# Attention, Fourier mixing and two feed-forward layers on one core: tables in 128 rows, another order of loads, cheaper transposes, and layer 1's last slots spread over fifteen chunks

## What is computed

```python
def phi(x):                                   # q, k: [4, 4, 1088, 32], S1, S2: [8, 32]
    a = einsum('rd,bhsd->bhsr', S1, x); b = einsum('rd,bhsd->bhsr', S2, x)
    return einsum('bhsi,bhsj->bhsij', a, b).reshape(..., 64)
kv, z = einsum('bhsf,bhsd->bhfd', phi(k), v), phi(k).sum(tokens)
x = (phi(q) @ kv) / (phi(q) @ z + 1e-6)       # -> [4, 1088, 128]
mixed = real(fft(fft(x, axis=tokens), axis=channels))
u = x + mixed
un = (u - mean(u)) / sqrt(var(u) + 1e-6)
x2 = u + relu(un @ w_ch1) @ w_ch2             # layer 1
h = relu(x2 @ w_in)                           # layer 2
conv = sum over k of conv_w[k] * h[token + k - 1]
out = (h * sigmoid(conv)) @ w_out
```

## Time and profile before

| | |
|---|---|
| median of 3 runs | 354.21 us (353.78 to 357.87) |
| span of the profiled execution | 352.7 us |
| PE busy | 312.0 us (88%) |
| DVE busy | 213.8 us (61%) |
| ACT busy | 191.6 us (54%) |
| POOL busy | 45.1 us (13%) |
| mean granted TensorE clock | 0.821 of full |
| DMA | 12.69 MB, mean 36 GB/s |

### The profile page before, as it was taken

One profiled execution on the slowest core, in us unless ns is written; L12 is line 12 of the kernel. 1 busy time (PEld: TensorE's weight loads), 2 busy tenths in 40 slices (PEclk: granted clock), 3 DMA queues, 4 the chain that ended last, 5 costly groups with the idle time before them and its releaser, 6 DMA issues.

```text
span 352.7 us, 4540 instructions
## 1 busy us (share of the span) xinstructions
PE 312.0 (88%) x1644; PEld 273.0 (77%) x1644; DVE 213.8 (61%) x373; ACT 191.6 (54%) x361; POOL 45.1 (13%) x93
## 2 busy tenths in 40 slices
PE   8499999999995019999998999979999899999966
PEld 7499999999995019989998987667876677878733
DVE  1522362233450004776888576948669999999994
ACT  2121023115211003556766798867778898999962
POOL 0000000008000001332222243830000000000000
PEclk9755555555555558999999999989999999999999
DMA  6800900200302000000000000000000100100101
GB/s 199 269 3 15 296 2 18 69 27 26 82 27 81 27 24 2 0 2 0 4 0 3 0 3 0 0 2 0 1 2 0 63 2 0 63 0 3 64 0 63
DMA packets 4192, 12.69 MB, mean 36 GB/s; under 512 B 780, under 2 KB 1548, under 8 KB 4170
## 3 DMA queue, kind: packets, MB, share of 16 engines
q1 hardware_dynamic: 4170, 12.41, 10.9%
HBM read 10.18 MB, written 2.23 MB: 35 GB/s over the span
## 4 chain that ended last, share of the span: by engine, by line
PE 29%; DVE 17%; ACT 4%; POOL 3%; issue 1%; POOLq 0%; DVEq 0%; ACTq 0%
PE ps L549 7%; DVE arena L945 5%; DVE arena L938 5%; DVE arena L933 5%; PE ps L460 5%; PE ps L462 5%; PE ps L461 5%; PE ps L453 3%; PE ps L503 2%; PE ps L509 2%; ACT arena L654 1%; PE ps L476 1%; ACT arena L740 1%; POOL arena L341 1%; ACT arena L727 1%
## 5 line engine op out<-in xcount | busy, mean ns | idle before, releaser
L549 PE MATMUL ps<-arena,wout 128*128 128x364 f32 (+1 forms) x192 | 63.6, 470 | 3.4 <-DVE arena L945 3.3
L549 PEld LDWEIGHTS ps<-arena,wout 128*128 128x128 f32 x192 | 35.5, 189 | 21.0 <-DVE arena L945 5.3
L933 DVE SCALAR_TENSOR_TENSOR arena<-arena,taps 128x1088 f32<-128x1088 f32 x32 | 43.1, 1348 | 5.6 <-ACT arena L735 5.5
L460 PE MATMUL ps<-x2hi,wlo 128*128 128x364 f32 x96 | 42.7, 445 | 4.1 <-ACT arena L727 2.9
L727 ACT ACTIVATE arena<-ps 128x364 f32<-128x364 f32 x96 | 40.7, 470 | 9.0 <-PE ps L462 8.8
L938 DVE SCALAR_TENSOR_TENSOR arena<-arena,taps 128x1088 f32<-128x1088 f32 x32 | 43.1, 1348 | 0.0
L945 DVE TENSOR_TENSOR arena<-arena 128x1088 f32<-128x1088 f32 (+2 forms) x36 | 41.4, 1162 | 1.2 <-ACT arena L740 1.2
L735 ACT ACTIVATE arena<-arena,taps 128x1088 f32<-128x1088 f32 x32 | 38.5, 1204 | 1.0
L740 ACT ACTIVATE arena<-arena 128x1088 f32<-128x1088 f32 x32 | 35.2, 1101 | 4.1 <-DVE arena L938 4.1
L798 DVE COPY arena<-ps 64x66 f32<-64x66 f32 x4 | 0.9, 220 | 58.0 <-PE ps L389 58.0
L389 PE MATMUL ps<-arena 121*128 121x66 f32 x144 | 32.7, 404 | 0.0
(11 more groups left out here) (82 smaller groups left out, 516.1 us busy)
## 6 DMA issues: line engine op xcount, KB each, us to landing
arena<-v_d SPq DMA_DIRECT2D x4, 561.5 KB
arena<-qT_d SPq DMA_DIRECT2D x4, 545.0 KB, 8.7
arena<-kT_d SPq DMA_DIRECT2D x3, 544.5 KB, 8.2
out_d<-arena SPq DMA_DIRECT2D x3, 544.0 KB, 2.7
cos_t<-cos_d SPq DMA_DIRECT2D x1, 789.0 KB
sin_t<-sin_d SPq DMA_DIRECT2D x1, 789.0 KB
wraw<-w_d SPq DMA_DIRECT2D x2, 256.0 KB, 6.2
wraw<-win_d SPq DMA_DIRECT2D x1, 512.0 KB, 7.3
```

The lines of the kernel that those rows point to most:

```text
L460: pe.matmul(out, lo, rhi, start=first, stop=False)
L549: pe.matmul(ps[:, OUT_BANK + t, 0:z - a], wout[:, c, :], gate[:, i % GATES, a:z], start=(c == 0), stop=(c == C2 - 1)).then_inc(wout_done, 1)
L933: dve.scalar_tensor_tensor(out=gate[:, i % GATES, 1:S + 1], in0=h2[:, i % HIDDENS, 0:S], scalar=taps[:, i % C2, 0:1], in1=gate[:, i % GATE ...
```

## The change

- `cos_t`, `sin_t` and the values get 128 rows (zeros below). `anti` is gone. `chan` is one table of 130 columns.
- SP's order: the first queries in two loads (`ld_half` for the first five tiles), then keys and queries of batch 1, values 0, identity and channel table, keys and queries of batch 2, weights, values 1, both token tables, keys and queries of batch 3, the rest.
- `mirror_fold` folds channels c and 128 - c as well, so `fold` has 5 tiles: two tensor operations of 640 elements and two of 315. Fold transposes fall from 10 to 5, spectra matmuls from 10 of 65 columns to 5 of 130.
- Rows whose tokens run backwards are turned by plain transposes, and x2 is written with a step of -2 or -1 (`token_range`).
- The residual is four transposes ahead of the row's first `down` (`is_transpose`, `start` at the first), and `res_done` is replaced by `w2_done`.
- Row transposes move from slot 1 of a row to slot 2, `normed_low` from slot 2 to 3, `mixed_low` of the first rows from 3 to 2.
- The remainders of the weights (`wlo`) are taken on VectorE (`weight_low`) and no longer on GpSimd.
- Batch 3's end is written out anew: token sums 1 after feature piece 3, row transposes 0 between attention pieces, slots 0 and 1 ahead of batch 3's fold transposes and slot 2 ahead of its spectra. Batch 3's spectra and fold transposes use banks 5 and 7.
- `FIRST_SLOTS` is 24 instead of 22, `MIX_STEPS` 15 instead of 12.

```diff
-MIX_STEPS = 12
+MIX_STEPS = 15
-ET_PIECES = [(0, 4), (4, 8), (8, 10)]
+ET_PIECES = [(0, 4), (4, 5)]
+SP_PIECES = [(0, 3), (3, 5)]
...
-        cos_t = sb("cos_t", [TQ, TABLES, TQ])
-        sin_t = sb("sin_t", [TQ, TABLES, TQ])
+        cos_t = sb("cos_t", [128, TABLES, TQ])
+        sin_t = sb("sin_t", [128, TABLES, TQ])
...
+        for n in range(2):
+            bank_of["folded", B - 1, n] = bank_of["spectra", B - 1, n] = (5, 7)[n]
-        FIRST_SLOTS = NC1 // 2 + 2
+        FIRST_SLOTS = NC1 // 2 + 4
...
-                sp.dma_start(qT[:, b % 2], qT_d[:, b, :]).then_inc(ld_q[b % 2], 16)
+                part = KQ_PIECES[2][2] * TQ if b == 0 else 0
+                if part:
+                    sp.dma_start(qT[:, 0, 0:part], qT_d[:, 0, 0:part]).then_inc(ld_half, 16)
+                sp.dma_start(qT[:, b % 2, part:], qT_d[:, b, part:]).then_inc(ld_q[b % 2], 16)
...
             load_sketched(0)
+            load_sketched(1)
+            load_values(0)
             sp.dma_start(ident[:], ident_d).then_inc(ld_ident, 16)
-            sp.dma_start(anti[:], anti_d).then_inc(ld_ident, 16)
             sp.dma_start(chan[:], chan_d).then_inc(ld_ident, 16)
-            load_values(0)
-            load_sketched(1)
             load_sketched(2)
-            load_values(1)
             sp.dma_start(wraw[:, 0:D1], w1_d).then_inc(ld_w, 16)
             sp.dma_start(wraw[:, D1:2 * D1], w2_d).then_inc(ld_w, 16)
             sp.dma_start(wraw[:, 2 * D1:], win_d).then_inc(ld_w, 16)
+            load_values(1)
+            sp.dma_start(cos_t[:], cos_d).then_inc(ld_tab, 16)
+            sp.dma_start(sin_t[:], sin_d).then_inc(ld_tab, 16)
             load_sketched(3)
-            load_values(2)
-            sp.dma_start(cos_t[:], cos_d).then_inc(ld_tab, 16)
-            load_values(3)
-            sp.dma_start(sin_t[:], sin_d).then_inc(ld_tab, 16)
             sp.dma_start(wout[:], wout_d).then_inc(ld_wout, 16)
             sp.dma_start(taps[:], cw_d).then_inc(ld_wout, 16)
+            load_values(2)
+            load_values(3)
...
-                    for j in range(NJ):
-                        mm = pe.matmul(ps[0:TQ, bank, j * L:(j + 1) * L], foldT[:, part * NJ + j, :], chan[:, part, :],
-                                       start=True, stop=True)
+                    for j in range(t0, t1):
+                        c = (j - t0) * 2 * L
+                        mm = pe.matmul(ps[0:TQ, bank, c:c + 2 * L], foldT[:, j, :], chan[:], start=True, stop=True)
...
-                        if not turned(r, side):
-                            mm = pe.transpose(out, un[:, side, b, :], ident[0:TQ, 0:TQ])
-                        else:
-                            mm = pe.matmul(out, un[:, side, b, :], anti[:], start=True, stop=True)
+                        mm = pe.transpose(out, un[:, side, b, :], ident[0:TQ, 0:TQ])
...
+                    for m in range(2 * BP):
+                        pe.matmul(ps[:, bank, m * TQ:(m + 1) * TQ], u[:, r % 4, m // BP, m % BP, :], ident[0:TQ, 0:TQ],
+                                  start=(m == 0), stop=False, is_transpose=True)
...
-                if c == C1 - 1:
-                    for side in range(2):
-                        for b in range(BP):
-                            m = side * BP + b
-                            mm = pe.matmul(ps[:, bank, m * TQ:(m + 1) * TQ], u[:, r % 4, side, b, :],
-                                           anti[:] if turned(r, side) else ident[0:TQ, 0:TQ], start=False, stop=(m == 2 * BP - 1))
-                    mm.then_inc(res_done, 1)
...
-                if c == 1 and r + 1 < NR:
+                if c == 2 and r + 1 < NR:
                     normed_transposes(r + 1)
...
+            for n in range(TR_PIECES):
+                features_and_values(B - 1, n)
+                if n == 2:
+                    token_sums(0)
+                if n == 3:
+                    token_sums(1)
+            fold_transposes(B - 2)
+            for n in range(len(AT_PIECES)):
+                attend(B - 1, n)
+                if n == 1:
+                    normed_transposes(0)
+            channel_spectra(B - 2)
+            token_sums(2)
+            pe.wait_ge(wlo_ready, 2)
+            slot(0)
+            slot(1)
+            fold_transposes(B - 1)
+            slot(2)
+            channel_spectra(B - 1)
...
+                dve.tensor_tensor(fold[:], here, there, ALU.add).then_inc(fold_step, 1)
+                dve.tensor_tensor(odd[:], here, there, ALU.subtract).then_inc(fold_step, 1)
+                dve.wait_ge(fold_step, 3 * b + 1)
+                dve.tensor_tensor(fold[:, :, 1:64], fold[:, :, 1:64], fold[:, :, 64:127], ALU.add).then_inc(fold_step, 1)
+                dve.wait_ge(fold_step, 3 * b + 3)
+                dve.tensor_tensor(fold[:, :, 64:127], odd[:, :, 1:64], odd[:, :, 64:127], ALU.subtract).then_inc(fold_ready, 1)
...
+                key_features(b + 1)
+                if b == 2:
+                    weight_low(0, 0, D1)
+                    weight_low(1, D1, 2 * D1)
                 block_diagonal(b)
+                query_features(b + 1)
                 normalise(b)
                 mirror_fold(b)
                 if b >= 1:
                     partner_fold(b - 1)
+            weight_low(2, 2 * D1, 2 * D1 + D2)
+            mixed_rows(0)
+            moments(0)
+            block_diagonal(B - 1)
+            mixed_rows(1)
             moments(1)
+            normalise(B - 1)
             normed_low(0)
+            mirror_fold(B - 1)
+            partner_fold(B - 2)
+            slot(0)
+            slot(1)
+            slot(2)
+            partner_fold(B - 1)
```

More of the change, by code:

```diff
@@ L142, in build @@
         rden = room(TQ, NQ, H)
-        fold = room(TQ, NQ, DM)
+        fold = room(TQ, NJ, DM)
+        odd = room(TQ, NJ, DM)
         warm = room(128, 256)
@@ L146, in build @@
         qphiT = room(128, 2 * NQ, TQ)
-        foldT = room(128, NQ, TQ)
-        spectra = room(TQ, 2, NJ - 1, L)
+        foldT = room(128, NJ, TQ)
+        spectra = room(TQ, NJ - 1, 2, L)
         used[0] = 0
@@ L695, in _ @@
             sketch_copies(1)
-            for b in range(B + 1):
-                if b < B:
-                    feature_copies(b)
-                else:
-                    normed_high(0)
-                    sine_copy(2)
+            for b in range(B - 1):
+                feature_copies(b)
                 if b >= 1:
                     fold_copies(b - 1)
-                if b == B - 1:
-                    sine_copy(1)
-                    normed_rows(0)
-                if b == B:
-                    slot(0)
                 if b + 2 < B:
@@ L748, in output @@
                     act.activation(outT[:, b % 2, a:z], ps[:, OUT_BANK + t, 0:z - a], ACT.Copy).then_inc(out_ready, 1)
-            for n in range(1, FIRST_SLOTS):
+            for n in range(3, FIRST_SLOTS):
                 slot(n)
@@ L823, in mirror_fold @@
             def mirror_fold(b):
+                here, there = x_nat[:, b, 0:NJ, :], x_nat[:, b, NJ:NQ, :]
                 dve.wait_ge(x_ready, len(AT_PIECES) * (b + 1))
@@ L996, in token_range @@
     first, last = int(tokens[keep[0]]), int(tokens[keep[-1]])
-    return slice(keep[0], keep[-1] + 1), (slice(q * BP, (q + 1) * BP), slice(1 + first, 1 + last + 1, step))
+    assert list(tokens[keep]) == list(range(first, last + (1 if step > 0 else -1), step))
+    return slice(keep[0], keep[-1] + 1), (slice(q * BP, (q + 1) * BP), slice(1 + first, 1 + last + (1 if step > 0 else -1), step))
 def kernel(q, k, v, S1, S2, moe_w_ch1, moe_w_ch2, moe2_w_in, moe2_conv_w, moe2_w_out):
@@ L1045 @@
                     values = np.where(out % 2 == parity, values, 0.0)
-                table[:, TABLE_OF[j] + n, :] = values
+                table[:TQ, TABLE_OF[j] + n, :] = values
     cos_t, sin_t = cos_t.astype(f), sin_t.astype(f)
```

151 lines of the change are left out of this document (73 added, 78 removed).

## The result

| | before | after |
|---|---|---|
| median | 355.34 us (353.78 to 357.87, 4 runs) | 285.13 us (284.65 to 285.63, 4 runs) |
| span of the profiled execution | 352.7 us | 282.8 us |
| PE, DVE busy | 312.0, 213.8 us | 256.7, 219.0 us |
| mean granted TensorE clock | 0.821 | 0.982 |

The ratio is 0.800, with a 95% interval of 0.795 to 0.805. The forecast was 273 in a range of 264 to 314: the direction and the size hold, and the point was 12 us too low. The likeliest case had a range of its own, 265 to 283, and the result lies 2 us above it.

What follows compares the result with a forecast made beforehand. Bounds: TensorE at half clock up to 103 us, a transfer up to 131, TensorE at full clock, then VectorE. Terms 67.0 + 9.3 + 8.3 + 36.4 + 71.6 + 70.9 + 7.7 = 271.2, plus 1.5: 273 us, range 264 to 314.

Steps and rivals of the forecast that it cites:

- The likeliest case: Whole kernel: full clock holds through attention, 273 us, own range 265 to 283, chance 0.53.
- The tables: Token tables before the first sums: 128 rows and earlier issue land them by about 30 to 40 us; 20.1 us stop goes.
- The start: Batch 0 and 1 sketches: keys land at 9.0 to 10.2, 5.0 us stop goes, attention starts at 13.8 instead of 21.9.
- 1.7 us more of lateness are needed before the stop is as long as the shortest that did: Wait for batch 1's keys: argument against the clock falling at the start, the shortest such stop being 2.1 us.
- Half clock does not end in attention: Attention of batches 0 to 2: its work ends neither half nor full clock; at full clock the stage takes 0.53 of its time.
- the clock falls in the first 13 us: Rival at the start: attention starts at 15 and runs at low clock, 106 us to batch 3's key-values, 312 in all; chance 0.22.
- It falls in batch 1 or 2: Rival in attention: 1 us stop behind ScalarE's weight copies at 46 drops the clock until the sums, +11, 284; chance 0.14.
- Steps up to layer 1: Start 13.8, batches 14.5, 16.1, 13.7, batch 3 to key-values 8.9, its rest 9.3, first slots 8.3, layer 1 36.4 us.
- After: 15 x 1.63 + 18 x 1.82 + 9.5 x 1.83 = 74.6, less the same 3.0: Layer 2's chunks mixed with 18 slots: TensorE's work gives 71.6 us, with VectorE then 13 of 15 chunks done.
- layer gain missing: Rival in both layers: rows late behind slot-later transposes, 36.4 becomes 41 and 71.6 becomes 79, 285; chance 0.06.
- That is covered: Layer 1, row transposes a slot later: copy and remainder fit within one slot and the sums; otherwise up to 1 us a row.
- There are two more slots: Layer 1 ahead of layer 2: 20 slots at 1.82 us make 36.4 against 36.8; 18 instead of 20 remain for layer 2.

Runs made afterwards that it cites:

- both load edits: Kernel before with both token tables in 128 rows and keys and queries of batch 1 issued right behind batch 0's: 328.95 us, ratio 0.922.
- the 6.5 us stop made on purpose: Changed kernel with keys and queries of batch 1 issued behind values 0, identity, channel table and batch 2's: 318.54 us, ratio 0.896.
- the load edits: Kernel before with token tables in 128 rows, keys of batch 1 first and values in 128 rows: 294.31 us (292.0 to 297.33), ratio 0.822.
- the best kernel: Changed kernel with 22 slots ahead of layer 2 and row transposes, their copy and remainder a slot earlier: 277.66 us, ratio 0.781.
- the start experiments: Kernel before with tables in 128 rows 334.04 us, batch 1's keys first 347.86, both 328.95, both plus values in 128 rows 294.31; changed kernel with keys late 318.54.

## Why the prediction was right, and where it wasn't

- **The tables: right.** Landing after 5.7 and 7.5 us, no stop; alone they bring 334.0 against 356.7 on the same chip, which is the 20 us of the wait within the spread of before (352.9 to 357.9).
- **The start: right in the time, with less room than I said.** The keys' stop is gone and attention starts at 13.4. But my step "1.7 us more of lateness are needed before the stop is as long as the shortest that did" took 2.1 us as the limit. 1.4 us was enough in the run with both load edits, and in after a 1.56 us stop (row 0, forecast as 1.4 us of wait without a price in clock) was followed by half clock from 70.3 to 73.7. What kept the full clock in attention was an edit I counted as nothing, the values in 128 rows: I had them land "by 13 to 16" and took the early end, and in the run without it they were waited for until 15.8.
- **Half clock does not end in attention: right for the old spectra**: 329 us with both load edits shows it. With the new ones it ended 1.2 us behind the first of them. The reading that it rose "during the first token sums" is wrong, they had ended 1.5 us before. My second case, "the clock falls in the first 13 us", was priced at 312 with low clock to the token sums. With the 6.5 us stop made on purpose it is 318.5; less that stop this gives about 312, an estimate, and it agrees by luck: the low clock ends earlier than the case has it, and attention starts later.
- **"It falls in batch 1 or 2": did not happen in after, happened in one execution of the kernel before with the load edits.** The place I named, ScalarE's weight copies, cost 0.5 us in after; the place where it fell there was TensorE's wait for VectorE, 1.37 us. The transposes in transpose mode are six more a row and not four (four residual ones, two of the row's four). They did not bring the clock down: it is 1.00 in the 39.0 us of layer 1. The Trainium skill ("TensorE: Matmul & The Clock Gate", Part 4: PE-mode transpose) says that transposes don't count as work for the clock; for a clock that is already full, beside layer 1's matmuls of 436 columns, this trace shows no harm from them.
- **Steps up to layer 1: right within 1.2 us each, layer 1 by 2.6.** The terms of the rest of batch 3 add up to 8.7 and not to the 9.3 taken; it measured 10.5. Rows stand 7.4 us apart, 1.86 a slot against my 1.82, so the transposes brought what I counted; the rest is one 1.5 us wait for a remainder at 117 and the last slots.
- **Layer 2: the step that failed is "After: 15 x 1.63 + 18 x 1.82 + 9.5 x 1.83 = 74.6, less the same 3.0".** It sums TensorE's work and takes the stops of before as the stops of after. The work was nearly as said (68.5 us busy), the stops were not: TensorE stood 11.5 of 80.0 us, most of it for relu, where before it stood 3.1 of 69.3. VectorE was said to be at chunk 13 after 71.6 us; it got there after 79.9. Before's trace had the mechanism: there too the last two roots took 7.7 and 10.9 us. Of my cases "layer gain missing" comes closest, with its late rows, its 79 for this stage and its 285; I gave it 0.06. But it had the rows late in the transposes and layer 1 at 41 (39.0 measured), so that its 285 is met to the tenth is luck.
- **"That is covered" for the transposes a slot later: wrong**, by 4.8 us, in layer 2 and not in layer 1 where I looked. **"There are two more slots" ahead of layer 2: wrong**, by 3.8 us: I moved their TensorE time and looked neither at VectorE's part of slot 25, which stands in front of the first tap, nor at where row 9 would fall among the chunks. Which of the two it was stays open.
- **Still open:** 4.5 us between the best kernel's span (275.7) and my 271.2; 1.2 of it is batch 3's rest, with the clock's fall behind row 0. And why after's clock stayed at 1.00 in 127 to 131, around a stop of 1.46 us, when 1.56 us at 68 brought it down.
- **Not tried:** the first queries in one load, and by themselves the removal of the flip matrix, the wider spectra, the cheaper transposes and the weight remainders on VectorE. Between the shorter executions with the load edits (292.0) and after lie 7 us that belong to these together.

## What to carry to other kernels

Time a stage by who waits for whom in program order, not by the busiest engine's work: a small chain on a side engine that a third engine's list waits for can hold two others. Before moving work ahead of a stage, look at what each engine then has in front of that stage's first instruction, and follow the gain through the stage: a lead of 4.7 us at the first tap was gone at the third. And when a stop is removed to save the clock, look for the next-latest arrival in the same place, since with a stop of 1.4 us the clock fell as with one of 5.

## What the runs showed of the hardware

- GpSimd's instructions on 109 x 4 elements took 0.2 us (the power 1.0) alone and 1.2 to 2.6 beside VectorE's taps, ending with VectorE's instructions; beside a VectorE read of PSUM they took 0.2 again. The other way round, VectorE's 109 x 2560 product, begun while GpSimd was at a weight remainder, took 4.17 us and 2.83 without; the 121 x 2304 product beside GpSimd's first remainder took the 2.55 us that it takes without, and there GpSimd's instruction was the longer one (3.8 us, where the next of the same 512 columns took 1.3). The Trainium skill ("SBUF — State Buffer", SBUF: two separate sides) has a pair of ports that VectorE with two SBUF inputs and GpSimd hold in turn, each for a whole instruction. The rows agree: the taps read two SBUF inputs, the remainder one and PSUM.
- With both load edits the clock stayed at half for 99 us (16.5 to 115.5), through attention with matmuls of 64 to 66 columns and hardly a gap, and through one group of token sums of 130 columns. Each rise out of it in before and the start experiments came 0.3 to 1.6 us behind the end of matmuls of 130 columns.
- With the row transposes, their copy and remainder a slot earlier, a 0.6 us instruction stands elsewhere between the taps; a GpSimd chain was 2.6 us shorter and the kernel 4.8.
